# The mask of the front parts moved ahead of their scores, two group sums moved to GpSimd, and a new order of the first stages

## The reference, cut to what matters

```python
# attention: batch 4, heads 8, seq 576, head_dim 64, factor 4
q_d = q.reshape(B, H, Sd, factor, D).mean(axis=3)       # Sd = 144; the same for k and v
out_d = softmax(scale * q_d @ k_d.T) @ v_d               # pooled attention
out_up = np.repeat(out_d, factor, axis=2)
mask = np.abs(pos[:, None] - pos[None, :]) < factor      # a band of +-3 positions
out_local = softmax(where(mask, scale * q @ k.T, -1e9)) @ v
x = (out_up + out_local)                                 # to (2304 tokens, 512)
h = max(x @ w1, x @ w2, x @ w3); y = h @ w_out           # 768 wide inside
g = leaky(y @ w_in); out = g @ w_out2                    # 2048 wide inside
```

## Time and profile before

| | |
|---|---|
| median of 3 runs | 772.26 us (772.16 to 773.0) |
| the profiled execution | 771.94 us, of which the span of the trace is 770.2 us |
| PE busy | 762.8 us, 99% |
| VectorE (DVE), ScalarE (ACT), GpSimd (POOL) busy | 446.5, 296.3, 167.0 us |

### The profile page before, as it was taken

One profiled execution on the slowest core, in us unless ns is written; L12 is line 12 of the kernel. 1 busy time (PEld: TensorE's weight loads), 2 busy tenths in 40 slices (PEclk: granted clock), 3 DMA queues, 4 the chain that ended last, 5 costly groups with the idle time before them and its releaser, 6 DMA issues.

```text
span 770.2 us, 13539 instructions
## 1 busy us (share of the span) xinstructions
PE 762.8 (99%) x5412; PEld 684.7 (89%) x5412; DVE 446.5 (58%) x769; ACT 296.3 (38%) x697; POOL 167.0 (22%) x208
## 2 busy tenths in 40 slices
PE   9999999999999999999999999999999999999998
PEld 7889989888888889999998988989898998889896
DVE  6867797666745463765756566564434466334433
ACT  4675544333242323433544354442222244222222
POOL 3795121211111333340435533110000000000000
PEclk9999999999999999999999999999999999999999
DMA  8642432332121023212567644446432236223402
GB/s 286 212 161 96 138 119 80 103 96 71 49 76 37 1 68 120 66 44 85 169 254 262 257 178 151 191 152 215 158 118 96 96 133 236 96 97 107 156 25 83
DMA packets 37630, 98.91 MB, mean 128 GB/s; under 512 B 2880, under 2 KB 23360, under 8 KB 34496
## 3 DMA queue, kind: packets, MB, share of 16 engines
q1 hardware_dynamic: 37568, 98.05, 36.4%
HBM read 73.92 MB, written 24.12 MB: 127 GB/s over the span
## 4 chain that ended last, share of the span: by engine, by line
PE 95%; DVE 2%; ACT 1%; issue 1%; DMA 1%; SPq 0%; DVEq 0%; ACTq 0%
PE mlp_ps L1067 10%; PE mlp_ps L1069 9%; PE mlp_ps L1068 9%; PE mlp_ps L1219 8%; PE mlp_ps L1221 8%; PE mlp_ps L1220 8%; PE att_ps L1240 6%; PE att_ps L1242 6%; PE att_ps L1241 6%; PE mlp_ps L1242 3%; PE mlp_ps L1241 3%; PE mlp_ps L1240 3%; PE att_ps L1139 2%; PE att_ps L1141 2%; PE att_ps L1140 2%; PE att_ps L1056 2%
## 5 line engine op out<-in xcount | busy, mean ns | idle before, releaser
L1067 PE MATMUL mlp_ps<-x_hi,wa_lo 128*128 128x288 f32 (+1 forms) x288 | 101.7, 353 | 0.1
L1069 PE MATMUL mlp_ps<-x_hi,wa_hi 128*128 128x288 f32 (+1 forms) x288 | 97.4, 338 | 0.0
L1068 PE MATMUL mlp_ps<-x_lo,wa_hi 128*128 128x288 f32 (+1 forms) x288 | 97.1, 337 | 0.0
L1507 ACT ACTIVATE h_last_a<-wa_raw 128x384 fp32r<-128x384 f32 x72 | 37.8, 524 | 104.7 <-DVE wa_raw L1841 104.1
L1067 PEld LDWEIGHTS mlp_ps<-x_hi,wa_lo 128*128 128x128 f32 x288 | 54.0, 188 | 6.0 <-DVE x_raw L1676 0.3
L1839 DVE TENSOR_TENSOR wa_raw<-mlp_ps,h_raw 128x384 f32<-128x384 f32 x24 | 13.4, 557 | 79.1 <-PE mlp_ps L1221 51.4
L1069 PEld LDWEIGHTS mlp_ps<-x_hi,wa_hi 128*128 128x128 f32 x288 | 54.1, 188 | 4.6
L1068 PEld LDWEIGHTS mlp_ps<-x_lo,wa_hi 128*128 128x128 f32 x288 | 54.3, 188 | 4.0
L1853 DVE TENSOR_TENSOR h_last_b<-wa_raw,h_last_a 128x384 fp32r<-128x384 f32 x72 | 43.3, 605 | 23.5 <-ACT h_last_a L1507 21.1
L855 POOL TENSOR_TENSOR v_rows<-v_rows 72x512 f32<-72x512 f32 x16 | 21.0, 1312 | 152.2 <-DMA v_rows<-in_v_sum 152.2
L1242 PE MATMUL att_ps<-wa_hi,h_last_a 128*128 128x512 f32 x132 | 52.2, 396 | 0.0
(11 more groups left out here) (215 smaller groups left out, 2049.1 us busy)
## 6 DMA issues: line engine op xcount, KB each, us to landing
u_even<-u_scratch SPq DMA_DIRECT2D x8, 1792.0 KB, 7.4
u_odd<-u_scratch SPq DMA_DIRECT2D x8, 1792.0 KB, 7.3
kq_in<-in_kq SPq DMA_DIRECT2D x14, 576.0 KB, 3.9
u_scratch<-u_even SPq DMA_DIRECT2D x4, 1792.0 KB, 8.7
u_scratch<-u_odd SPq DMA_DIRECT2D x4, 1792.0 KB, 9.7
v_rows<-in_v_sum SPq DMA_DIRECT2D x16, 288.0 KB
wa_raw<-in_w SPq DMA_DIRECT2D x6, 768.0 KB, 6.3
v_win<-in_v_band SPq DMA_DIRECT2D x12, 384.0 KB, 3.6
```

The lines of the kernel that those rows point to most:

```text
L1067: nc.tensor.matmul(ps, wlo, xhi, start=(n == 0), stop=False)
L1068: nc.tensor.matmul(ps, whi, xlo, start=False, stop=False)
L1069: last = nc.tensor.matmul(ps, whi, xhi, start=False, stop=(n == len(pairs) - 1))
L1507: nc.scalar.activation(g_tile(0, quad, part), g_raw[part], ACT.Copy).then_inc(g_hi_ready, 1)
```

## The change

Three edits are made, all before the MLP runs at full rate.

1. The mask of the front parts is copied once by ScalarE into float32r (`front_mask`, with a float32r `ident_r`, both in the memory of `h_hi`). The two mask matmuls then run in float32r and *ahead* of the local scores, before the wait for keys and queries. The local scores end the accumulation.
2. The group sums D of pairs 2 and 3 move from VectorE to GpSimd, in two additions each over a scratch area in `wo_raw`. The load of chunk 6 waits for them.
3. The list in `first_phase()` is written anew. All FRONT units run local scores before pooled scores; unit 0 takes its local maxima, shift and exponentials before the pooled ones; fewer zero matmuls are issued; W, G, N, T, E and LR/WL items of units 0 to 5 stand in other places.

```diff
+POOL_SUMS = (2, 3)
...
+        ("LR", 2), ("WL", 1), ("LR", 3),
+        ("Z", 8), ("D", 0), ("S", 0), ("E", 0), ("D", 1), ("G", 0), ("D", 2), ("Z", 2), ("N", 0), ("S", 1), ("E", 1), ("G", 1),
+        ("Z", 4), ("T", 0), ("S", 2), ("E", 2), ("N", 1), ("D", 3), ("V", 0), ("LV", 2), ("XH", 0, 0), ("W", 0, 0),
...
-    for c, at in ((2, 0.5), (3, 2.4), (4, 5.4), (5, 8.4)):
+    put(1.5, ("W", 2, 1))
+    for c, at in ((3, 2.4), (4, 5.4), (5, 8.4)):
...
-    return kinds[2:] + kinds[:2] if item[:2] in (("S", 0), ("S", 1)) else kinds
+    return kinds[2:] + kinds[:2] if item[0] == "S" and UNITS[item[1]][1] == FRONT else kinds
...
+            def group_sums(u):
+                p = UNITS[u][0]
+                pool.wait_ge(kq_loaded[p % PAIRS], 16 * (p // PAIRS + 1))
+                n = SD + sum(PART_GROUPS[FRONT][0])
+                src = kq_of(p).rearrange("p x s -> p (x s)")[:, 0:FACTOR * n].rearrange("p (a f) -> p a f", f=FACTOR)
+                twos = wo_raw[:, 0:2 * n].rearrange("p (f a) -> p f a", f=2)
+                nc.gpsimd.tensor_tensor(twos.rearrange("p f a -> p a f"), src[:, :, 0:2], src[:, :, 2:4], ALU.add).then_inc(kq_part, 1)
+                nc.gpsimd.tensor_tensor(kq_sum[:, p % PAIRS, 0:n], twos[:, 0, :], twos[:, 1, :], ALU.add).then_inc(sums_pooled, 1)
...
+                if part == FRONT:
+                    if u == 0:
+                        pe.wait_ge(mask_high, 2)
+                    for h in range(2):
+                        nc.tensor.matmul(ps[h][:, 0:(hi - lo) * TQ], ident_r, front_mask[:, h, :], start=True, stop=False)
+                pe.wait_ge(kq_loaded[p % PAIRS], 16 * (p // PAIRS + 1))
...
-                                         mask[:, SLOTS // 2 * h + lo:SLOTS // 2 * h + hi, :].rearrange("p s w -> p (s w)"),
-                                         start=False, stop=True).then_inc(att_done, 1)
```

More of the change, by code:

```diff
@@ L455, in build @@
         pool_step = sem("pool_step")
+        mask_high = sem("mask_high")
+        kq_part = sem("kq_part")
+        sums_pooled = sem("sums_pooled")
         mask_ready = sem("mask_ready")
@@ L545, in evacuation @@
                 "sl1": (shifted, u + 1) if part == FRONT else (masked, u + 1 - PAIRS),
-                "sg0": (exp_done, 2 * u + 1),
-                "sg1": (exp_done, 2 * u + 1),
+                "sg0": (exp_done, 2 * u + 1 if u else 2),
+                "sg1": (exp_done, 2 * u + 1 if u else 2),
                 "dt0": (probT_evac, EVACS[u] + 1),
@@ L693, in weights @@
             def weights(c):
+                if c == NF1:
+                    sp.wait_ge(sums_pooled, len(POOL_SUMS))
                 src = w123[c] if c < NF1 else w_out[(c - NF1) * P:(c - NF1 + 1) * P, :]
@@ L913, in _ @@
                     sums(item[1])
+                elif item[0] == "D" and item[1] in POOL_SUMS:
+                    group_sums(item[1])
                 elif item[0] == "W":
@@ L957, in local_scores @@
                                                 q[rows, Q_START[t]:Q_START[t] + TQ], k[rows, W_START[t]:W_START[t] + TQ],
-                                                start=(part != FRONT or t < 2), stop=(part != FRONT))
-                        if t == blocks[-1] and part != FRONT:
+                                                start=(part != FRONT), stop=(part != FRONT or t in blocks[-2:]))
+                        if t == blocks[-1]:
                             last.then_inc(att_done, 1)
[L961 to L967, removed]
-                                         mask[:, SLOTS // 2 * h + lo:SLOTS // 2 * h + hi, :].rearrange("p s w -> p (s w)"),
-                                         start=False, stop=True).then_inc(att_done, 1)
             def pooled_scores(u):
                 p, part = UNITS[u]
-                pe.wait_ge(sums_ready, u + 1)
+                if u in POOL_SUMS:
+                    pe.wait_ge(sums_pooled, POOL_SUMS.index(u) + 1)
+                else:
+                    pe.wait_ge(sums_ready, u + 1 - sum(i < u for i in POOL_SUMS))
                 begin(("sg0", u))
@@ L1268, in exps, with local_exps @@
                 nq, ng = tiles[0][1], len(tiles)
+                def local_exps():
+                    act.wait_ge(shifted, u + 1)
+                    local = prob_l[:, u % 2, 0:n, :]
+                    nc.scalar.activation(local, local, ACT.Exp, scale=SCALE).then_inc(exp_done, 1)
+                if u == 0:
+                    local_exps()
                 act.wait_ge(max_ready, u + 1)
+                if part == FRONT and u >= 2:
+                    act.wait_ge(att_done, JOB["dt0", u - 2] + 1)
                 nc.scalar.activation(bias_g[:nq, u % 2, 0:2 * ng], row_max[:nq, SLOTS:SLOTS + 2 * ng], ACT.Copy,
@@ L1279, in exps @@
                 last.then_inc(exp_done, 1)
-                act.wait_ge(shifted, u + 1)
-                local = prob_l[:, u % 2, 0:n, :]
-                nc.scalar.activation(local, local, ACT.Exp, scale=SCALE).then_inc(exp_done, 1)
+                if u:
+                    local_exps()
             def normalise(u):
@@ L1453, in _ @@
             nc.scalar.activation(table_loader[:, :], table_loader[:, :], ACT.Exp)
+            act.wait_ge(pool_step, 3)
+            nc.scalar.activation(ident_r, ident[:, :], ACT.Copy).then_inc(mask_high, 1)
+            act.wait_ge(mask_ready, 3)
+            m0, m1 = PART_MASK[FRONT]
+            nc.scalar.activation(front_mask.rearrange("p h (s w) -> p h s w", w=TQ),
+                                 mask[:, :, :].rearrange("p (h s) w -> p h s w", h=2)[:, :, m0:m1, :], ACT.Copy).then_inc(mask_high, 1)
             for item in FIRST:
@@ L1621, in shifts @@
                                         ALU.subtract).then_inc(shifted, 1)
+                if u == 0:
+                    pooled_maxima()
             def normalise(u):
@@ L1802, in _ @@
             for item in FIRST:
-                if item[0] == "D":
+                if item[0] == "D" and item[1] not in POOL_SUMS:
                     group_sums(item[1])
```

25 lines of the change are left out of this document (16 added, 9 removed), and 13 rows, old and new, of the table items.

## The result

The changed kernel takes 779.23 us (median of 4 runs, 778.65 to 779.58), the kernel before 772.21 us in the same session (4 runs, 771.74 to 773.0): a ratio of 1.009, 95% interval 1.0077 to 1.0103. The direction was forecast, the size was not: +7.0 us instead of +2.25, and outside the range of 772.9 to 777.0. The profiled execution has a span of 777.2 us, +7.0 against the 770.2 of before.

The account below looks back on a forecast made before the run. Up to about 26 us a relay between DVE, ScalarE and PE sets the pace, then PE's dense queue. Terms 0.5 + 0.4 + 1.15 + 0.2 = +2.25 us gave 774.5 us, range 772.9 to 777.0.

Parts of the forecast that it names:

- First MLP matmul: PE's start of the MLP: 26.6 instead of 26.06 us, waiting for GpSimd's low weight parts; +0.5, bounds -0.1 and +1.1.
- the relay: DVE, ScalarE and PE handing work on until about 26 us; first half of weight chunk 0 done at 19.3 us.
- my middle: GpSimd's low parts of chunk 0 ahead of the MLP: 7.1 to 7.4 us, with 7.2 used in the sum.
- V of unit 3: Comes +4.8 us behind the first MLP matmul instead of 4.41, behind later copies of T; +0.4, from 0.2 to 0.6.
- a sign that I would be right: PE waiting some 3 us for GpSimd's `wa_lo` ahead of a first MLP matmul at 26.3 to 27 us.
- Group 3: Its passes wait for low parts of chunk 1, +4.1 to +4.3 us behind V of unit 3; +1.15, from 0.9 to 1.25.
- S of unit 6: Waits for ScalarE's copy of T, giving back the 0.76 us gained at T of unit 4; +0.2, from -0.5 to +0.6.
- GpSimd's sums: Two additions on GpSimd, 1.17 and 0.67 us, done at 12.2 before PE wants them at 13.1; no cost taken.
- The mask: Two float32r mask matmuls take 0.25 us; 0.85 us leaves the path of unit 0, 0.6 that of units 1 to 3.
- The rivals: Smaller stalls behind the start (0.19), GpSimd's strided sums costing twice or more (0.17), a faster MLP start (0.08).
- the third: MLP starts as soon as attention lets it; 771.5 us, or 770.4 with group 3 not stalling; chance 0.08.
- my cap of 23.6: Earliest first MLP matmul under the faster start, since chunk 0's low parts were ready at 23.49; gain at most 2.5 us.

Follow-up runs that it names:

- its experiment: Changed kernel with 10 zero matmuls instead of 4 ahead of T of unit 0, nothing else; 778.95 us, ratio 1.0087 to the kernel before.
- The gap experiment: Kernel with the new front and the old list behind it, GpSimd waiting for its own previous low part (chunks 0 and 1); 773.1 us, ratio 1.0012.
- the new front: Changed kernel, chunk 0's weights early, 10 zeros ahead of T of unit 0; old order from V of unit 2, chunk 1 ahead of T3; 774.61 us.

## Why the prediction was off, step by step

- **First MLP matmul (forecast +0.5, was +2.86): the step that failed is the relay.** I laid rows end to end that were taken at full clock and with DVE held no longer than in the kernel before. N of unit 0 came out at 1.90 us and took 3.28 (+1.4, DVE's hold). The clock's first fall is worth about 0.9 of the 1.15 us of its experiment: there N of unit 0 was 0.4 us shorter by a shorter hold (1.79 us for the second multiplication, 0.18 for the first) and began 0.2 us later. That is from one execution. GpSimd's chain of low parts was 0.4 us longer than my middle. These make 2.7, less 0.2 for an earlier `row_sum` (8.49, not 8.72): 2.5, against 2.4 missed.
- **V of unit 3 (forecast +0.4, was +2.92): the copies behind `x_hi` of unit 2 were sized rightly**, as 4.84 and 4.85 us at full clock show against my 4.8. The missing 2.5 us are the clock's second fall. I had read the wait of some 3 us for `wa_lo` as a wait and nothing more, and had even listed it as a sign that I would be right; I never asked what PE's clock would do behind it. The zeros that the change leaves out stood in my sum with nothing, without a reason.
- **Group 3 (+1.15, was +1.22) and S of unit 6 (+0.2, was +0.13)** came as worked out. All five kernels with the new order of chunk 1's halves and no held `x_lo` (the changed one; it with zeros in both waits, in the first, in the second; and it without GpSimd's sums) show the same wait of 1.14 to 1.17 us for `wa_lo` ahead of group 3, and of 1.13 to 1.15 us for the copies of T ahead of S of unit 6; none with the old list does.
- **The mask.** 0.36 us for a pair of mask matmuls instead of my 0.25, so 0.49 us less for a unit and not 0.6; 0.9 us of it reach the MLP in the old order. In the changed kernel it can't be seen at the total.
- **GpSimd's sums.** I asked what the additions cost GpSimd, bounded that from 1.8 to 5.6 us, and it was 1.66. I did not ask what they cost DVE. That was the dear side.
- **The rivals.** None of mine named the clock. The early MLP of the third can be had: with both halves of chunk 0 early it starts at 23.78 to 24.65, near my cap of 23.6. It does not pay, since DVE is held later; and where the gap undoes that hold, the low parts come too late for group 3.

Two holes stay. The gap experiment shows what holds `x_lo`; why GpSimd's low parts are lengthened for DVE in the kernel before, where they also stand back to back (4.98 us for eight), and hold it for five in a row behind the new front, no run tells. And the exact moment at which the clock falls is not settled: with nearly the same wait ahead of T of unit 0 (1.54 and 1.65 us) it fell at about 12 us in the changed kernel and between 14 and 15 us in the one with zeros in the second wait alone; and behind a wait of 1.67 us ahead of V of unit 1 it fell at 24 us with zeros in both waits, and not there with zeros in the first alone.

No version here gains by the new order. The kernel before with the new mask alone, at 0.9987 (0.9978 to 0.9996), is the only one that beats both, by 0.1%.

## What to carry to other kernels

When a change makes PE wait, price the wait twice: its length, and all that follows at half the clock; here 3.63 us of standing still cost 2.5 us more behind it. Work that only fills waits, as the zeros here, belongs in the sum as a part that is removed. And when work moves to GpSimd, look on DVE for what runs beside it: instructions that read two operands from SBUF, or a small `tensor_scalar`, can wait through several GpSimd instructions that follow each other without a pause.

## What was unexpected in the hardware

- DVE can lose its turn to GpSimd many times in a row: 3.17, 3.26 and 3.26 us for a subtraction of 0.46, while GpSimd's low parts beside them, all but the last, ran at their own pace of 0.58 us. A wait of GpSimd for its own last instruction (0.11 us for each) gave DVE its turn (0.64 us). The Trainium skill (SBUF — State Buffer, Who interferes with whom) says that a DVE instruction with two SBUF inputs contends with GpSimd's reads, that a `tensor_scalar` can take the shared ports, and that the loser fully blocks. The trace agrees that instructions of both kinds are held beside GpSimd; that the port is what holds them, it does not show. The 128x14 multiplication of 1.20 to 1.66 us in six kernels, 0.17 alone, shows that a DVE instruction need not be large to be held for over a microsecond.
- GpSimd's addition with pairs read out of groups of four, 462 columns, took 0.98 to 1.02 us, less than the 1.17 that I worked out from the plain sums. The Trainium skill (GPSIMD Engine Reference, Performance pitfalls for Q7 kernels) has a read with a step of more than 8 bytes cost half as much again, and asks that the inner step be 8 bytes at most. The 1.75 us that I estimated by it, with the 16 bytes from pair to pair as the step, did not come. The inner step of this read is 4 bytes, within a pair, so the rule need not reach it, and the rule itself is not tested here.
- With the clock at 0.50, PE's matmuls of 288 columns followed each other 0.24 us apart (29.30 to 30.98), where they are 0.13 us apart at 1.00.
